# The last two tiles' recurrence outputs: four quarters of 32 columns in place of two halves of 64

## The reference, cut to what matters

```python
for t in range(S):
    m_new = np.maximum(f_gate[:, :, t] + m, i_gate[:, :, t])
    f_stab, i_stab = np.exp(f_gate[:, :, t] + m - m_new), np.exp(i_gate[:, :, t] - m_new)
    m = m_new
    C = f_stab[:, :, None, None] * C + i_stab[:, :, None, None] * np.einsum('bhd,bhe->bhde', vt, kt)
    n = f_stab[:, :, None] * n + i_stab[:, :, None] * kt
    h_tilde = np.einsum('bhde,bhe->bhd', C, qt)
    denom = np.maximum(np.abs(np.einsum('bhd,bhd->bh', n, qt)[:, :, None]), 1.0)
    y[:, :, t] = 1.0 / (1.0 + np.exp(-o_gate[:, :, t])) * h_tilde / denom
# x = y as (tokens, heads * 40)
# layer 1: (sigmoid(x @ w_gate) * (x @ w_val)) @ w_out
# layer 2: x / rms * rms_g, then (silu(x @ w_gate2) * (x @ w_val2)) @ w_out2
```

## Time and profile before

| | |
|---|---|
| time before, median of 3 runs | 448.56 us (448.35 to 449.09) |
| the profiled execution's own time | 448.17 us |
| its span in the profile | 446.3 us |
| TensorE matmul busy | 441.9 us, 99% of the span |
| TensorE weight loads busy | 404.1 us, 91% |
| VectorE, ScalarE, GpSimd busy | 216.0, 183.9, 88.9 us |
| chain that ended last | TensorE 98% |
| line L1164 in that chain | 3% |
| mean granted TensorE clock | 1.000 of full speed |

### The profile page before, as it was taken

How to read it: one execution, slowest core, us unless ns; L and a number is a source line. 1 busy time by engine, 2 the same in 40 slices (tenths; PEclk the granted TensorE clock), 3 DMA queues, 4 the chain that set the end, 5 groups by cost and what they waited for, 6 DMA issues and landing times.

```text
span 446.3 us, 10769 instructions
## 1 busy us (share of the span) xinstructions
PE 441.9 (99%) x4573; PEld 404.1 (91%) x4574; DVE 216.0 (48%) x481; ACT 183.9 (41%) x358; POOL 88.9 (20%) x138
## 2 busy tenths in 40 slices
PE   8999999999999999999999999999999999999997
PEld 5899999999999999988889988889988899888897
DVE  6876937854556456423432237561065630256510
ACT  7885377534663473124553144231033320233310
POOL 4567810112110200004556190000000000000000
PEclk9999999999999999999999999999999999999999
DMA  8984600331232114001333010000000000000000
GB/s 235 304 282 142 181 1 3 91 89 30 64 91 75 38 39 160 1 2 40 120 114 125 3 46 1 1 0 31 31 1 1 1 16 29 17 1 0 1 31 29
DMA packets 12032, 27.55 MB, mean 62 GB/s; under 512 B 1824, under 2 KB 6208, under 8 KB 11984
## 3 DMA queue, kind: packets, MB, share of 16 engines
q1 hardware_dynamic: 11728, 26.80, 19.7%
q10 hardware_dynamic: 256, 0.07, 0.1%
HBM read 24.81 MB, written 1.97 MB: 60 GB/s over the span
## 4 chain that ended last, share of the span: by engine, by line
PE 98%; DMA 1%; SPq 0%; ACT 0%; issue 0%
PE bank L1275 37%; PE bank L1226 21%; PE bank L1294 10%; PE bank L1296 9%; PE bank L1295 9%; PE bank L1164 3%; PE bank L1127 2%; PE bank L1047 2%; PE bank L1146 1%; PE bank L1083 1%; PE bank L1173 1%; DMA step<-in_qk_t 1%; PE bank L1114 0%; PE bank L1306 0%; PE bank L1321 0%; PE bank L1329 0%
## 5 line engine op out<-in xcount | busy, mean ns | idle before, releaser
L1275 PE MATMUL bank<-x_hi,wgv_hi 64*128 64x512 f32 x576 | 105.8, 388 | 0.0
L715 ACT ACTIVATE sg<-bank 128x256 f32<-128x256 f32 (+1 forms) x96 | 47.1, 492 | 128.6 <-PE bank L1275 82.6
L1275 PE MATMUL bank<-x_lo,wgv_hi 64*128 64x512 f32 x480 | 93.9, 386 | 0.0
L997 DVE TENSOR_TENSOR bank<-sg,bank 128x256 f32<-128x256 f32 (+1 forms) x96 | 53.8, 560 | 57.5 <-ACT sg L715 55.8
L1226 PE MATMUL bank<-x_hi,wgv_hi 128*128 128x256 f32 x288 | 80.6, 290 | 0.0
L1226 PE MATMUL bank<-x_lo,wgv_hi 128*128 128x256 f32 x288 | 77.8, 282 | 0.0
L1294 PE MATMUL bank<-wo_hi,h_hi 128*128 128x320 f32 x240 | 75.3, 314 | 0.0
L1275 PE MATMUL bank<-x_hi,wgv_lo 64*128 64x512 f32 x384 | 75.1, 386 | 0.0
L1296 PE MATMUL bank<-wo_hi,h_lo 128*128 128x320 f32 x240 | 74.1, 309 | 0.0
L1295 PE MATMUL bank<-wo_lo,h_hi 128*128 128x320 f32 x240 | 74.1, 309 | 0.0
L995 DVE TENSOR_TENSOR sg<-sg,bank 128x512 f32<-128x512 f32 x36 | 24.8, 688 | 83.0 <-ACT sg L715 83.0
(11 more groups left out here) (152 smaller groups left out, 554.8 us busy)
## 6 DMA issues: line engine op xcount, KB each, us to landing
step<-in_qk_t SPq DMA_DIRECT2D x24, 192.0 KB, 3.9
step<-in_vok SPq DMA_DIRECT2D x12, 324.0 KB, 4.2
step<-in_w_gv SPq DMA_DIRECT2D x6, 576.0 KB, 3.8
raw_x<-in_w_gv SPq DMA_DIRECT2D x4, 576.0 KB, 7.8
raw_p<-in_w_gv SPq DMA_DIRECT2D x4, 576.0 KB, 6.6
step<-in_vok SPq DMA_DIRECT2D x10, 160.0 KB, 5.7
raw_p<-in_w_o SPq DMA_DIRECT2D x3, 480.0 KB, 3.2
y<-y_tok SPq DMA_DIRECT2D x9, 160.0 KB, 1.8
```

Of the source, the lines that this page charges most:

```text
L715: act.activation(sg_view(n), g_view(n), ACT.Sigmoid).then_inc(sg_done, 1)
L997: dve.tensor_tensor(v_view(n), sg_view(n), v_view(n), ALU.mult).then_inc(hf_done, 1)
L1275: mm = pe.matmul(ps(n), w, x, start=own and (s, p) == (0, 0), stop=last and not own)
```

## The change: quarters for tiles 10 and 11

For the tiles in `BY_QUARTERS` (10 and 11) the N piece's slices are 32 queries wide instead of 64. Each head then has four matmuls, one on each group of 32 of TensorE's columns, instead of two. The first two quarters take the values that the first half took, the last two those of the second half. Operands, results, waits and the increment at the end of the piece are the same.

```diff
+BY_QUARTERS = [NT - 2, NT - 1]
@@ piece "N"
+                    w = Q if n in BY_QUARTERS else HALF
                     for i in range(2):
                         pe.wait_ge(p_done, 2 * n + i + 1)
                         for c in range(HG):
@@
-                            for u in range(2):
-                                us = slice(HALF * u, HALF * u + HALF)
+                            for u in range(P // w):
+                                us = slice(w * u, w * u + w)
                                 mm = pe.matmul(bank[base(n) + 2][us, h * D1:(h + 1) * D1], wexp[b][:, h, us],
-                                               values[u], start=True, stop=True)
+                                               values[w * u // HALF], start=True, stop=True)
```

## The result

| | before | changed |
|---|---|---|
| median, 20 runs each | 448.53 us (448.18 to 449.09) | 448.00 us (447.48 to 448.40) |
| ratio, 95% interval | | 0.9987 (0.9981 to 0.9993) |
| profiled execution: span | 446.3 us | 446.3 us |

The kernel became faster by 0.13%, some 0.6 us (0.53 by the medians). That is within the 0.2% that the prediction counted as no change, but clear of zero. The forecast was 448.0. That it was met to the digit is luck: single runs of either kernel spread over 0.9 us.

What follows compares the result with a forecast made beforehand. TensorE's own stream, busy 99% of the span, was taken as the bound. Two pieces gaining 0.28 us each made 0.56 us, 448.56 to 448.00 us; the terms' ends gave 447.9 to 448.2, the stated range 447.3 to 449.2 us.

Steps and rivals of the forecast that it cites:

- The bound: Whole kernel: TensorE, busy 99%, passes gains in tiles 10 and 11's N to the end one for one; ceiling 2.13 us.
- The round: Tiles 10 and 11's N: sixteen rounds stay, each falling from 58 ns, set by loading 64 weight columns, to 38 ns.
- The piece: Each N piece of tiles 10 and 11: first to last start 0.62 us against 0.90, gain 0.28 us.
- 1: N pieces: two quarters of a half share one load path, rounds stay 58 ns, 448.6 us; 0.19 with the sequencer rival.
- 3: N pieces: only two of four quarters stream at once, rounds of 76 ns, 449.1 us; chance 0.07.
- 4: N pieces: no load runs under a matmul, rounds of 84 ns, 449.4 us; chance 0.02.
- 2, the sequencer: N pieces: TensorE fed no faster than 14 ns a matmul, 0.90 us as now, 448.6 us; 0.19 with the two-load-paths rival.
- The fetching of instructions: Whole kernel: 64 more loads and 64 more matmuls, their fetching taken as hidden under 0.12 us matmuls; cost nothing.
- What follows: Behind tiles 10 and 11's N: VectorE begins earlier, TensorE's margins of 2.3 and 4.1 us stay, no wait added.

Runs made afterwards that it cites:

- e5: Changed kernel with halves again in all tiles, and only 20 of 41 moving columns in tiles 10 and 11's N pieces; 448.15 us, one run.
- e7: Changed kernel with each head in tiles 10 and 11's N as one matmul over all 128 queries; 449.59 us, one run.
- e3: Changed kernel with tiles 10 and 11's N ordered quarter by quarter within each group of four heads; 449.80 us, 1.0023 of the kernel before.
- e6: Changed kernel with the I piece of tiles 10 and 11 in quarters too; 450.12 us, 1.0037 of the kernel before.
- e1: Changed kernel with quarters in the N pieces of all twelve tiles; 451.38 us, 1.0057 of the kernel before.
- e2: Changed kernel with N in quarters in tiles 0, 1, 10 and 11; 453.22 us, 1.0096 of the kernel before.
- e8: Changed kernel with N in quarters in tiles 2 to 11; 450.07 us, 1.0031 of the kernel before.
- e9: Changed kernel with N in quarters in tiles 0 and 2 to 11; 451.38 us, 1.0051 of the kernel before.
- e12: Changed kernel with N quarters in tiles 2 to 11 and 128 set-semaphore tests before layer 1 matmuls; 447.11 us, 0.9972 of the kernel before.
- e11: Changed kernel plus 40 set-semaphore tests before layer 1 matmuls, quarters still in tiles 10 and 11; 447.94 us, 0.9986 of the kernel before.

## Why the prediction was right

- **The bound.** TensorE's stream sets the end, one for one. Right: 0.62 us less in the two pieces, 0.62 less from there to the end in the profiled execution and within 0.03 us of that in seven more traces, and 0.13% (0.3 to 0.9 us) in the runs.
- **The round.** Sixteen rounds stay and the load of 64 columns is their price. Shown: moving columns don't matter with halves (e5), width does (e7). The forecast put 38 ns. Most rounds take 36, the stream's 41 columns, as a lone tile shows too (e3); the thirteen behind the first two lie between 35 and 40, 37 in the mean.
- **The piece.** 0.62 us forecast, 0.622 measured, and here two small errors cancel. The first two rounds take 53 and 49 ns, 28 ns above two of the mean, and 30 were put down for that. Fifteen rounds at 37 ns are 16 ns less than forecast. But the last four starts spread over 40 ns, where 20 were put down: they no longer come close together as at the start. The gap behind the last start was taken as 0.16 us and is 0.128; it follows the last weights and moving columns (0.142 with halves of 20 moving columns, 0.116 with quarters of 20). So each piece gained 0.31 us and not 0.28, and the sum is 0.62 and not 0.56, within its stated ends.
- **The rivals.** 1 and 3 (two load paths, two streams) are refuted by the four starts within 0.02 us at rounds of 36 ns. 4 is refuted by the same. 2, the sequencer at 14 ns a matmul, is refuted: 64 matmuls in 0.622 us are 9.9 ns each. But a limit of this kind isn't far away: in e6 eight tiles got no further than 9 ns.
- **The fetching of instructions.** Costed at nothing with one sentence, "hidden now under matmuls of 0.12 us each before and behind". True for tiles 10 and 11 as placed, by 0.5 to 0.8 us: the tightest block was used 3.0 us after its transfer began, where 2.2 to 2.5 are needed. It was the weakest step of the working. The prediction sends whoever doubts it to its second rival, but that one prices a matmul every 14 ns, and not a stall; none of the four rivals stands for what happened in the experiments. The theories of e1, e2 and e8 left it out too (e8 had it as a rival), and failed by 3.5 to 5.2 us on it. The slower rival with a price and a place would have been this one.
- **What follows.** No wait appeared behind T10 or T11. VectorE starts on tile 11 with 0.19 us of idle time in front instead of the 0.51 in the earlier trace rows:

```profile
179.25 0.56 DVE L888 TENSOR_TENSOR inter<-bank,ecol 128x164 f32<-128x164 f32 x2 [0.19 <-PE bank L1167]
```

Open: what sets the start of a block's transfer, and why it and the time from there to the block's use vary. It wasn't tried.

## What to carry to other kernels

When small matmuls on column tiles follow each other on other weights, the round in these kernels is the longer of the weight columns' load and the moving columns' stream, so halving the columns pays until the two are equal, and only if the tiles' matmuls stand next to each other in the stream. Count what it does to the instruction stream too: a stretch that uses more than 256 loads and matmuls in under about 2.5 us can run dry, and whether it does depends on where the blocks of 256 fall, so a change elsewhere in the kernel can move a stall of 0.4 to 3.6 us in or out. The longer ones were followed by some microseconds of the lower clock, so the loss is more than the wait. When a wait is put down to "issue", look at the instruction queue's transfers before looking for a data dependence.

## What the hardware showed that I had not expected

- TensorE's instructions arrive in transfers of 16384 bytes; each stall stood at a recorded number 449 + 256 k and ended 2.2 to 2.8 us after its transfer began.
- Eight tiles of 40 rows by 32 columns go at 9 ns a matmul, slower in all than four of 64 columns (0.58 us against 0.45 for the same work).
- Behind stalls of 3.5 us (e1, e2), 2.3 us (e9) and 1.5 us (e6) TensorE was granted 1.2 GHz for 6.8, 6.8, 3.4 and 3.4 us; behind those of 1.6 us (e12), 1.3 us (the first of e9) and 0.4 to 0.6 us (e8) it kept 2.4 GHz.
- A test of a set semaphore shows no cost where one stands in front of a matmul of 120 ns (e11, 40 of them); where four stand in front of three matmuls it is 16 ns each (2.1 us for 128).
